# Bucketed attention and two gated layers on one core: where the match work of the next pair stands, and the set-up of the first pair

## The reference

```python
q_bits = (np.einsum('bhsd,dk->bhsk', q, proj) > 0).astype(np.int64)
k_bits = (np.einsum('bhsd,dk->bhsk', k, proj) > 0).astype(np.int64)
q_bucket = np.sum(q_bits * powers, axis=-1)
k_bucket = np.sum(k_bits * powers, axis=-1)
mask = q_bucket[:, :, :, None] == k_bucket[:, :, None, :]
scores = scale * np.matmul(q, k.transpose(0, 1, 3, 2))
scores = np.where(mask, scores, -1000000000.0)
```

## Time and profile before

| what | value |
|---|---|
| median of 3 runs | 512.54 us |
| the profiled execution | 510.61 us, of which span 508.8 us |
| PE busy | 481.3 us (95%) |
| DVE, ACT, POOL busy | 354.3, 283.4, 271.1 us |
| granted TensorE clock, mean | 0.999 |
| share of the chain that ended last: PE, DVE, issue, ACT | 70%, 15%, 7%, 6% |

### The profile page before, as it was taken

How to read it: one execution, slowest core, us unless ns; L and a number is a source line. 1 busy time by engine, 2 the same in 40 slices (tenths; PEclk the granted TensorE clock), 3 DMA queues, 4 the chain that set the end, 5 groups by cost and what they waited for, 6 DMA issues and landing times.

```text
span 508.8 us, 9512 instructions
## 1 busy us (share of the span) xinstructions
PE 481.3 (95%) x3564; PEld 408.0 (80%) x3564; DVE 354.3 (70%) x604; ACT 283.4 (56%) x601; POOL 271.1 (53%) x259
## 2 busy tenths in 40 slices
PE   8679989999899998999999999999999999999997
PEld 7556666666566665666777999999999999999997
DVE  3676697796978969788858798597398298325211
ACT  3696776868768687786664543354245145144140
POOL 5693663936549274494136674548247347445240
PEclk9999999999999999999999999999999999999999
DMA  5121030311202112020022000100000100100101
GB/s 197 32 82 49 11 119 17 100 47 41 89 17 100 47 60 72 16 68 17 17 84 84 1 2 1 43 1 12 31 2 2 43 1 1 43 0 2 43 2 43
DMA packets 10575, 20.83 MB, mean 41 GB/s; under 512 B 1696, under 2 KB 6816, under 8 KB 10528
## 3 DMA queue, kind: packets, MB, share of 16 engines
q1 hardware_dynamic: 10224, 19.94, 11.9%
q10 hardware_dynamic: 304, 0.27, 0.2%
HBM read 17.06 MB, written 3.15 MB: 40 GB/s over the span
## 4 chain that ended last, share of the span: by engine, by line
PE 70%; DVE 15%; issue 7%; ACT 6%; POOL 2%; DMA 1%; DVEq 0%; ACTq 0%; POOLq 0%
PE ps L679 27%; PE ps L687 11%; PE ps L667 11%; PE ps L629 10%; PE ps L643 8%; ACT q L440 3%; DVE negmax L803 3%; DVE gate L846 3%; DVE pt L810 2%; DVE k L795 1%; DVE tmp_a L916 1%; DMA raw_q<-qT 1%; PE ps L604 1%; ACT probs L448 1%; DVE tmp_b L914 1%
## 5 line engine op out<-in xcount | busy, mean ns | idle before, releaser
L803 DVE TENSOR_REDUCE negmax<-ps 128x1 f32<-128x768 f32 x96 | 91.8, 956 | 48.6 <-PE ps L629 47.8
L629 PE MATMUL ps<-k,q 128*128 128x384 f32 x384 | 92.2, 362 | 12.5 <-ACT probs L448 12.0
L448 ACT ACTIVATE probs<-ps,negmax 128x768 f32<-128x768 f32 x96 | 86.6, 902 | 17.2 <-DVE negmax L803 15.4
L643 PE MATMUL ps<-ident,probs 128*128 128x128 f32 x576 | 82.2, 275 | 4.4 <-DVE pt L810 4.1
L629 PEld LDWEIGHTS ps<-k,q 128*128 128x128 f32 x384 | 63.0, 189 | 28.0 <-ACT probs L448 22.8
L643 PEld LDWEIGHTS ps<-ident,probs 128*128 128x128 f32 x576 | 67.0, 140 | 14.2 <-DVE pt L810 5.5
L667 PE MATMUL ps<-pt,vals 128*64 128x384 f32 x384 | 68.8, 494 | 0.8 <-DVE x L836 0.8
L456 ACT ACTIVATE pt<-ps 128x384 f32<-128x384 f32 x96 | 46.7, 487 | 31.0 <-PE ps L643 28.8
L406 POOL TENSOR_TENSOR h_lo<-tmp_b,h_hi 128x256 fp32r<-128x256 f32 x48 | 38.5, 807 | 46.0 <-ACT h_hi L546 46.0
L846 DVE SCALAR_TENSOR_TENSOR gate<-x,conv_sb,gate 128x256 f32<-128x256 f32 x96 | 60.9, 634 | 2.4
L810 DVE COPY pt<-ps 128x384 f32<-128x384 f32 x96 | 52.2, 544 | 3.5 <-PE ps L643 3.5
(11 more groups left out here) (88 smaller groups left out, 1161.5 us busy)
## 6 DMA issues: line engine op xcount, KB each, us to landing
w_raw<-w SPq DMA_DIRECT2D x8, 640.0 KB, 4.0
raw_q<-qT SPq DMA_DIRECT2D x8, 384.0 KB, 3.0
raw_k<-kT SPq DMA_DIRECT2D x8, 384.0 KB, 4.4
vals<-v SPq DMA_DIRECT2D x16, 192.0 KB, 2.3
out<-w_raw SPq DMA_DIRECT2D x24, 128.0 KB, 1.7
...
proj_bd<-proj ACTq DMA_DIRECT2D x2, 1.5 KB, 3.9
```

Of the source, the lines that this page charges most:

```text
L448: act.activation(probs[par][:, :], score[par], ACT.Exp, bias=negmax[:, t:t + 1], accum_out=sums[:, t, 0:1]).then_inc(exp_done, 1)
L629: last = pe.matmul(ps[:, 2 * par + half, 0:HALF], qq[h][:, q], kk[h][:, half * HALF:(half + 1) * HALF], start=first, stop=not first)
L643: last = pe.transpose(tbank[u][:, k * P:(k + 1) * P], probs[g % 2][:, kt * P:(kt + 1) * P], ident[:, :])
L803: dve.tensor_reduce(negmax[:, t:t + 1], score[g % 2], AX.XY, ALU.max, negate=True).then_inc(max_done, 1)
```

## The change

1. **Matches go by head.** Match j = 0 holds the queries of head A for both halves of the tokens, 1 the keys of head A, 2 and 3 those of head B. The table `codes` is laid out for that on the host, as 16-bit words, and is read straight into `codes_b`; POOL's cast of it is gone.
2. **Places.** For pair p > 1, project, bits_out and match 0 stand at t = 11 of pair p - 2, match 1 at t = 2 of pair p - 1 ahead of the product, match 2 at t = 5 ahead of the product and match 3 behind it. ACT's pieces stand at t = 11 and 5, DVE's at t = 2 and 8, behind the taps. For pair 1 the old places stay.
3. **Taps.** In pairs 2 to 7 two stand at t = 2; t = 8 keeps two; t = 11 keeps two.
4. **Queries.** `raw_q` has two buffers. DVE scales it in place (`scale_queries`, 128x768) right behind bits_out; POOL's scaling and `q_eighth` are gone. ACT's high queries of head A stand both at t = 2 (one ahead of `reciprocals_up`, one behind) and those of head B both at t = 8. POOL subtracts the low queries of head B last.
5. **Set-up.** One transfer for the projection, laid out on the host; 18, 5 and 14 transposes in place of 32, 8 and 20; head B's high queries and keys ahead of its one-hot pieces and of the first maximum; the first two matmuls of a head's first score don't wait for the low queries.

The core of the diff:

```diff
+
+
+FIRST_MATCH = {2: 0, 4: 1, 5: 2, 7: 3}
+FIRST_HOTQ, FIRST_HOTK = {3: 0, 6: 1}, {5: 0, 8: 1}
+MATCH_AHEAD, MATCH_BEHIND = {2: 1, 5: 2}, {5: 3}
+HOTK_STEPS = {2: 0, 8: 1}
 
 SETS = 3
...
 
 
 
+    if i > 1 and t == 2:
+        return range(6 * (i - 1) - 2, 6 * (i - 1))
     if i == PAIRS - 1:
         return {5: range(36, 38), 8: range(38, 40)}.get(t, ())
-    if i and t == 8:
-        return range(6 * (i - 1), 6 * (i - 1) + 2)
-    if i and t == 11:
-        return range(6 * (i - 1) + 2, 6 * i)
+    if i and t in (8, 11):
+        first = 6 * (i - 1) + (t == 11) * 2
+        return range(first, first + 2)
     return ()
 
...
-                wait(sp, qhi_done, 4 * p)
-                wait(sp, qscaled, p)
-                wait(sp, bits_mm, p)
-                sp.dma_start(raw_q[:, :], qT[p, :, :]).then_inc(q_in, 16)
+                wait(sp, qhi_done, 4 * (p - 1))
+                wait(sp, qlo_done, 2 * (p - 1))
+                wait(sp, bits_mm, p - 1)
+                wait(sp, q_in, 16 * p)
+                sp.dma_start(raw_q[p % 2][:, :], qT[p, :, :]).then_inc(q_in, 16)
 
             def load_k(p):
...
         def _(pool):
-            def scale_queries(p):
-                pool.wait_ge(q_in, 16 * (p + 1))
-                wait(pool, qlo_done, 2 * p)
-                pool.tensor_scalar(q_eighth[:, :], raw_q[:, :], DH ** -0.5, None, ALU.mult).then_inc(qscaled, 1)
...
                                base=0, pattern=[[-1, P]], channel_multiplier=1).then_inc(ident_up, 1)
-            scale_queries(0)
-            pool.wait_ge(codes_in, 16)
-            pool.tensor_copy(codes_b[:, :, :], codes_f[:, :, :]).then_inc(codes_up, 1)
-
-            pool.wait_ge(codes_up, 1)
+
+            pool.wait_ge(ident_up, 1)
             for head in range(2):
                 low_keys(head)
                 low_queries(head)
...
                 if i < LAST:
-                    scale_queries(i + 1)
+                    if i:
+                        pool.wait_ge(rcpw_done, 2 * i)
...
                     pool.wait_ge(rcpw_done, 2 * i + 1)
-                    low_queries(2 * i + 3)
                     high_keys(2 * i + 3)
                     low_keys(2 * i + 3)
+                    low_queries(2 * i + 3)
                     pool.wait_ge(klo_done, 2 * i + 4)
+                    pool.wait_ge(qlo_done, 2 * i + 4)
 
             def w2_low(n):
...
                 act.activation(gate[:, c % 2, :, :], gate[:, c % 2, :, :], ACT.Tanh, scale=0.5).then_inc(tanh_done, 1)
 
-            act.wait_ge(proj_zero, 1)
-            act.dma_start(proj_bd[LO, 0:BITS], proj).then_inc(proj_in, 16)
-            act.dma_start(proj_bd[HI, BITS:2 * BITS], proj).then_inc(proj_in, 16)
-            act.dma_start(codes_f[:, :, :], codes).then_inc(codes_in, 16)
+            act.dma_start(proj_bd[:, :], proj).then_inc(proj_in, 16)
+            act.dma_start(codes_b[:, :, :].bitcast(U16), codes).then_inc(codes_in, 16)
             high_queries(0, 0)
             high_queries(0, 1)
             act.wait_ge(two_up, 1)
-            hot_queries(0, 0, A)
-            hot_queries(0, 1, A)
-            hot_queries(0, 0, B)
-            hot_queries(0, 1, B)
-            exp_tile(0)
+            hot_queries(0, A)
             high_queries(1, 0)
             high_queries(1, 1)
+            hot_queries(0, B)
+            exp_tile(0)
             for g in range(PAIRS * TILES):
                 i, t = divmod(g, TILES)
                 head, tt = divmod(g, KT)
...
+                    hot_queries(i + 1, B)
                 if g + 2 < PAIRS * TILES and product_step(g):
                     exp_tile(g + 2)
+                if t == 2 and 0 < i < LAST:
+                    high_queries(2 * i + 2, 0)
+                if t == 8 and 0 < i < LAST:
+                    high_queries(2 * i + 3, 0)
                 if tt == R_STEP and head:
                     reciprocals_up(head - 1)
-                if i < LAST:
-                    if t in HOTQ_STEPS:
-                        for h in range(2):
-                            hot_queries(i + 1, HOTQ_STEPS[t], h)
+                if t == 11 and i + 2 < PAIRS:
+                    hot_queries(i + 2, A)
+                if i == 0:
+                    if t in FIRST_HOTQ:
+                        hot_queries(1, FIRST_HOTQ[t])
                     if t == 2:
-                        high_queries(2 * i + 2, 0)
+                        high_queries(2, 0)
                     if t == 5:
+                        high_queries(2, 1)
+                        high_queries(3, 0)
+                    if t == 8:
+                        high_queries(3, 1)
+                elif i < LAST:
+                    if t == 2:
                         high_queries(2 * i + 2, 1)
-                        high_queries(2 * i + 3, 0)
                     if t == 8:
                         high_queries(2 * i + 3, 1)
                 else:
...
-                    pe.wait_ge(hotq_up, hot_count(head))
-                    pe.wait_ge(hotk_up, hot_count(head))
+                    pe.wait_ge(hotq_up, 2 * (head + 1))
+                    pe.wait_ge(hotk_up, 2 * (head + 1))
                 wait(pe, exp_done, g - 1)
                 q = slice(tq * P, (tq + 1) * P)
                 for qq, kk, first in ((q1, k1, True), (q2, k2, False)):
+                    if tq == 0 and not first:
+                        pe.wait_ge(qlo_done, head + 1)
                     for half in range(2):
                         last = pe.matmul(ps[:, 2 * par + half, 0:HALF], qq[h][:, q],
...
-            pe.wait_ge(proj_in, 32)
+            keep_busy(18)
+            pe.wait_ge(proj_in, 16)
             project(0)
-            keep_busy(8)
-            pe.wait_ge(codes_up, 1)
-            for j in (0, 1, 3, 2):
+            keep_busy(5)
+            pe.wait_ge(codes_in, 16)
+            for j in range(4):
                 match(0, j)
-            keep_busy(20)
+            keep_busy(14)
             scores(0)
             scores(1)
...
                 transposes(g)
+                if t == TILES - 1 and i + 2 < PAIRS:
+                    project(i + 2)
+                if 0 < i < LAST and t in MATCH_AHEAD:
+                    match(i + 1, MATCH_AHEAD[t])
                 if tt in PV_STEPS and head:
                     product(head - 1, PV_STEPS[tt])
                 if tt == R_STEP and head:
                     spread(head - 1)
-                if i < LAST:
+                if t == TILES - 1 and i + 2 < PAIRS:
+                    match(i + 2, 0)
+                if 0 < i < LAST and t in MATCH_BEHIND:
+                    match(i + 1, MATCH_BEHIND[t])
+                if i == 0:
                     if t == 1:
-                        project(i + 1)
-                    if t in MATCH_STEPS:
-                        match(i + 1, MATCH_STEPS[t])
-                elif t >= TILES - 2:
+                        project(1)
+                    if t in FIRST_MATCH:
+                        match(1, FIRST_MATCH[t])
+                if i == LAST and t >= TILES - 2:
                     pe.wait_ge(xlo_done, 1)
                     s_val_tile(0, 2 * (t % 2))
...
-                    .then_inc(hotk_up, 1)
+            def scale_queries(p):
+
+                dve.wait_ge(q_in, 16 * (p + 1))
+                if p:
+                    dve.wait_ge(bits_mm, p + 1)
+                dve.tensor_scalar(raw_q[p % 2][:, :], raw_q[p % 2][:, :], DH ** -0.5, None, ALU.mult)\
+                    .then_inc(qscaled, 1)
+
+            def hot_keys(p, h):
+                dve.wait_ge(cnt_mm, 4 * p + 2 * h + 2)
+                wait(dve, s_done, KT * (2 * p + h - SETS + 1))
+                for half, rows in enumerate((LO, HI)):
+                    dve.tensor_scalar(k1[(2 * p + h) % SETS][LO, half * HALF:(half + 1) * HALF],
+                                      match_bank(p, 2 * h + 1)[rows, :], 2.5, -FAR, ALU.is_lt, ALU.mult)\
+                        .then_inc(hotk_up, 1)
 
             def tile_max(g):
...
 
-            dve.memset(proj_bd[:, :], 0.0).then_inc(proj_zero, 1)
             dve.memset(neg_two[:, :], -2.0).then_inc(two_up, 1)
             dve.memset(sums[:, :, 1:2], 1e-9).then_inc(eps_up, 1)
             dve.memset(x[:, :, 0:HALO], 0.0).then_inc(halo_up, 1)
+            scale_queries(0)
             high_keys(0)
             bits_out(0)
-            hot_keys(0, 0, A)
-            hot_keys(0, 1, A)
-            hot_keys(0, 0, B)
-            hot_keys(0, 1, B)
+            hot_keys(0, A)
+            high_keys(1)
+            hot_keys(0, B)
             tile_max(0)
-            high_keys(1)
             tile_max(1)
             for g in range(PAIRS * TILES):
...
                 second_half_up(g)
-                if i < LAST:
+                if i == 0:
                     if t == 2:
-                        bits_out(i + 1)
-                    if t in HOTK_STEPS:
-                        for h in range(2):
-                            hot_keys(i + 1, HOTK_STEPS[t], h)
+                        bits_out(1)
```

(8 more changed lines are left out.)

82 lines of the change are left out of this document (35 added, 47 removed).

## The result

| | before | after |
|---|---|---|
| median of 4 runs each | 512.51 us | 505.84 us |
| lowest and highest | 510.19, 512.74 | 504.81, 507.09 |
| profiled execution, span | 510.61, 508.8 us | 506.26, 504.5 us |

What follows compares the result with a forecast made beforehand. ACT was taken to bound steps 2 to 7 and DVE steps 8 to 10. Pairs' 6.4 us plus 1.4 from set-up and pair 0 made 7.8 off 512.54: 504.7 us, range 501 to 510.5.

Steps and rivals of the forecast that it cites:

- What bounds: Within a pair, ACT bounds steps 2 to 7 and DVE steps 8 to 10, by PE's waits of 0.68 and 0.74 us.
- Steps 2 to 7: Exponential 1.0 us sooner; product of step 2 to 5 takes 7.2 us (was 8.03), 5 to 8 takes 7.4 (was 7.87).
- Steps 8 to 10: DVE's first tap waits for POOL's instruction to end; step 11's product comes 23.3 us after step 2's, against 23.93.
- Rival A: POOL and step 8's taps miss each other: 0.7 us more in pairs 2 to 5, 0.2 in 1 and 6; 501.5; 15%.
- Rival B: At step 8 POOL's low queries precede the second tap, holding it 1.82 us; pairs 2 to 4, 5.4 us, 510.1; 20%.
- Line 843's tap runs at once: At step 8 of pairs 1 and 6 the first tap reads one tensor and doesn't wait for POOL: 0.5 us more gain.
- pair 7 costs nothing: Pair 7's two taps at step 2 lie in the same hole of 2.2 us, without keys: no gain or loss.
- Pairs 5 and 6: Gains of 0.9 us in pair 5, whose second tap is line 843's, and 1.8 in pair 6, without projection.
- Set-up and pair 0: First maximum at 12.0, exponential 2 at about 16.05, 2.5 us sooner; net gain 1.4 us, bounds 0 and 3.5.
- rival D: Fewer warming transposes leave PE at 1.2 GHz through head 0, costing 9.8 us in all: 514.5; 7%.
- Scaling on DVE: The 128x768 scaling takes 0.58 us; in pair 0's step 2, ACT's wait for bits_out and scaling loses 0.5 us.

Runs made afterwards that it cites:

- Experiment 1: Changed kernel with the two taps of step 8 of pairs 1 to 6 moved to step 11, making four there; 499.59 us, ratio 0.979.
- Experiment 4: Changed kernel with 20 more warming transposes behind score 1 and 14 more ahead of pair 0's match 2 at step 5; 506.21 us, ratio 0.991.
- experiment 2: Changed kernel with POOL's low queries of head B waiting for DVE's one-hot keys of step 8; 505.72 us, ratio 0.991.
- experiment 6: Changed kernel with POOL's low queries waiting for DVE's step 8 keys, plus pair 7's two taps moved from step 2 to 5; 503.57 us, ratio 0.986.
- 9: Changed kernel with POOL's low queries waiting for DVE's step 8 keys, plus the old 32, 8 and 20 warming transposes; 505.38 us, ratio 0.990.
- experiment 3: Changed kernel with POOL's low queries waiting for DVE's step 8 keys, plus pair 1's queries scaled at step 0 of pair 0; 504.04 us, ratio 0.987.
- 8: Changed kernel with step 8 taps at 11, early scaling for pair 1, more warming transposes and pair 7's taps at step 5; 496.46 us, ratio 0.973.

## Why the prediction was right, and where not

- **What bounds (right).** ACT in steps 2 to 7, DVE in 8 to 10. With ACT's pieces moved, PE's waits for exponentials are gone from its rows, and those for DVE are left.
- **Steps 2 to 7 (right).** 7.20 and 7.30 us for a forecast of 7.2 and 7.4, in all six pairs. The exponential came 1.0 sooner, as forecast. The 0.2 for a match is what 7.20 has above pair 7's 6.97 of before; in steps 5 to 7 it was less, 7.30 for 7.23.
- **Steps 8 to 10 (mechanism right, one pair on the rival's side).** 8.7 was forecast; 8.61 came in pairs 3 and 4, 8.47 and 8.36 in 1 and 5. A tap waits until POOL's instruction ends. Experiment 1, where it is 7.86 (7.06 in pair 6), shows the whole price: 0.5 to 0.75 us in a pair and 2.6 in pair 2. Rival A had put it at 0.7 in pairs 2 to 5, which is about right, pair 2 apart, and at 0.2 in pairs 1 and 6, where it was 0.6.
- **Rival B (true in pair 2 alone, in both traces of the changed kernel and in that of 4).** The prediction gave POOL's low queries 0.15 us of leeway and called it against B. Pair 2 has POOL's chain start 0.36 us later than pairs 3 and 4, and that was enough: the row "0.16 <-ACT" at 99.27 is this margin. It cost 1.8 us in the trace against pairs 3 and 4, and 1.6 more where the clock fell after it; experiment 2, which takes away this order alone, won 1.5 of the 1.8 back. A forecast by a margin that is smaller than the step to the next pair should have priced one or two pairs at B, and not all or none. B's own price for a caught pair (1.8) was right. Why POOL starts later in pair 2 stays open.
- **Line 843's tap runs at once, and pair 7 costs nothing (wrong).** The tap took 1.16 us for 0.35 at step 8 of pairs 1 and 6, and 2.47 in pair 7. There the prediction had put both taps of step 2 "in the same hole" as in the other pairs. But in pairs 2 to 6 POOL sleeps at that place, since its low queries wait for ACT, and pair 7 has no low queries: POOL splits weights and x, and both taps wait for it. That cost 1.3 us, and experiment 6 won it back. The trace of before had such a wait of line 843, in pair 5, on DVE:

```profile
195.44 1.93 DVE L843 TENSOR_SCALAR gate<-x,conv_sb 128x256 f32<-128x256 f32 x1
```

  Its median over 24 is 0.346 us, so this one waited 1.6 for POOL's low keys. The Trainium skill (SBUF — State Buffer, "Who interferes with whom") lists copy, cast and tensor_scalar among what may take the port shared with GpSimd, when their operands meet its conditions, and I had used only its part on two inputs; the trace agrees, with 0.35 us alone and 2.47 beside POOL. "Pair 7: nothing" is the term that was mis-sized.
- **Pairs 5 and 6.** 1.23 and 1.62 for 0.9 and 1.8, so the terms are off by 0.3 and 0.2. In pair 5 line 843's tap is the second of step 8 and did run at once (0.34 us), since POOL was idle by then; in pair 6 it is the first and waited.
- **Set-up and pair 0 (the work about right, the clock missed).** The first maximum came at 12.03 for 12.0, in part by luck: the keys were taken to be there at about 4.8 and came at 5.24, and from there it was 6.8 us where the prediction had 7.2. In the nine traces of this set-up the first maximum starts anywhere from 11.97 to 13.31. Exponential 4 was no sooner in the trace (23.63 for 23.60) where 1.2 was forecast. Experiment 4, with the clock full, gives 1.25 there and 1.76 at S2 of pair 1 for 1.4. So the term was about right at full clock, and the clock costs some 2 us of it. That is rival D in mechanism: with more transposes (4), or the old number of them (9), the clock stayed full in pair 0 in the executions traced. But it is not D in place: the low clock doesn't last through head 0, it comes twice for 3 to 4 us, after waits of 2.4 and 1.9 us. D's price of 9.8 us was five times too high.
- **Scaling on DVE.** 0.56 us, forecast 0.58; experiment 3, and 8 beside 4, put the wait that it makes in pair 0 at 0.6, where 0.5 was charged.
- **The total.** 504.7 forecast, 505.8 measured. In the profiled execution 4.1 to 4.35 us of the 7.8 came; missing are 1.5 of pair 2, 1.4 of pair 0 and 1.3 of pair 7, less 0.6 that the other pairs gave beyond their terms. The medians are 2.3 us further apart, because the median of before lay 1.9 above its profiled execution and that of after 0.4 below; the forecast had carried the 1.9 over to after. In the experiments the kernel before gave 510.3 to 510.4, so the 1.9 was no lasting property of it. That the total came so near is in good part luck.
